# Weight pieces five to eight of the first batch rounded later, behind the copies of the last attention unit

## The reference

```python
state = alpha_t * state + k_t v_t^T;  y_t = q_t state         # 8 heads of 48, 768 tokens
x = y                                                        # 4 x 768 x 384
u = x + (x^T @ U @ V)^T                                      # rank 32
x = u + relu(u @ w_ch1) @ w_ch2                              # 384 -> 1536 -> 384
theta = x @ w_theta
u = x + w_tok_r @ (x * cos(theta)) + w_tok_i @ (x * sin(theta))
out = u + relu(u @ w_ch)
```

## Time and profile before

| what | us |
| --- | --- |
| median of three runs | 663.69 (663.62 to 664.41) |
| the profiled execution's own time | 664.45 |
| its span in the trace | 662.7 |
| busy in the span: TensorE | 651.1 |
| VectorE | 324.8 |
| ScalarE | 262.9 |
| GpSimd | 255.8 |

### The profile page before, as it was taken

One profiled execution on the slowest core, in us unless ns is written; L12 is line 12 of the kernel. 1 busy time (PEld: TensorE's weight loads), 2 busy tenths in 40 slices (PEclk: granted clock), 3 DMA queues, 4 the chain that ended last, 5 costly groups with the idle time before them and its releaser, 6 DMA issues.

```text
span 662.7 us, 15705 instructions
## 1 busy us (share of the span) xinstructions
PE 651.1 (98%) x6380; PEld 627.3 (95%) x6380; DVE 324.8 (49%) x543; ACT 262.9 (40%) x542; POOL 255.8 (39%) x250
## 2 busy tenths in 40 slices
PE   9979999999999999999999999999999999999998
PEld 5769999999999999999999999999999999999998
DVE  8938774255564255663242115765425543444522
ACT  5855544234544233544233334434324421432320
POOL 6757852133323133332112562347314531733220
PEclk9979999999999999999999999999999999999999
DMA  9466202006103015110004350220041023002101
GB/s 318 140 269 236 94 32 99 2 29 233 47 3 127 2 47 216 47 36 4 2 36 181 106 162 17 73 84 25 12 136 66 0 65 125 24 0 83 60 1 71
DMA packets 25163, 54.84 MB, mean 83 GB/s; under 512 B 2193, under 2 KB 17041, under 8 KB 25105
## 3 DMA queue, kind: packets, MB, share of 16 engines
q1 hardware_dynamic: 25104, 53.99, 23.4%
HBM read 44.55 MB, written 9.44 MB: 81 GB/s over the span
## 4 chain that ended last, share of the span: by engine, by line
PE 94%; DVE 2%; ACT 2%; issue 1%; DMA 1%; ACTq 0%; DVEq 0%
PE banks L774 24%; PE banks L804 22%; PE banks L1169 21%; PE banks L1241 6%; PE banks L1087 5%; PE banks L404 3%; PE banks L1144 2%; PE banks L525 2%; PE banks L465 2%; PE banks L533 2%; PE banks L719 1%; PE banks L1555 1%; DVE tokiL L247 1%; DMA stage<-w 1%; PE banks L724 1%
## 5 line engine op out<-in xcount | busy, mean ns | idle before, releaser
L788 DVE SCALAR_TENSOR_TENSOR hidL<-banks,hidH 128x384 fp32r<-128x384 f32 x96 | 53.4, 556 | 121.4 <-ACT hidH L784 121.0
L774 PE MATMUL banks<-uH,w1H 128*128 128x384 f32 x288 | 100.0, 347 | 0.3 <-ACT uH L751 0.3
L804 PE MATMUL banks<-hidH,w2H 128*128 128x384 f32 x288 | 96.6, 335 | 0.4 <-ACT x_nat L645 0.2
L774 PE MATMUL banks<-uH,w1L 128*128 128x384 f32 x288 | 96.5, 335 | 0.0
L804 PE MATMUL banks<-hidH,w2L 128*128 128x384 f32 x288 | 96.5, 335 | 0.0
L774 PE MATMUL banks<-uL,w1H 128*128 128x384 f32 x288 | 96.5, 336 | 0.0
L804 PE MATMUL banks<-hidL,w2H 128*128 128x384 f32 x288 | 96.2, 334 | 0.0
L784 ACT ACTIVATE hidH<-banks 128x384 fp32r<-128x384 f32 x96 | 47.0, 490 | 86.0 <-PE banks L774 86.0
L1227 POOL TENSOR_TENSOR u2L<-x_res,u2H 128x384 fp32r<-128x384 f32 x24 | 24.5, 1020 | 95.8 <-ACT u2H L1221 95.8
L390 POOL TENSOR_TENSOR k_end<-qka_sb,tail 112x384 f32<-112x384 f32 x32 | 31.5, 983 | 68.2 <-DVE tail L353 65.0
L774 PEld LDWEIGHTS banks<-uH,w1H 128*128 128x128 f32 x288 | 54.1, 188 | 2.5 <-issue 0.6
(11 more groups left out here) (134 smaller groups left out, 1416.4 us busy)
## 6 DMA issues: line engine op xcount, KB each, us to landing
qka_sb<-qka SPq DMA_DIRECT2D x28, 582.5 KB, 6.6
v_sb<-v_nat SPq DMA_DIRECT2D x32, 144.0 KB, 6.1
stage<-w SPq DMA_DIRECT2D x6, 768.0 KB, 5.2
x_dram<-u_t SPq DMA_DIRECT2D x8, 576.0 KB, 3.8
x_f<-x_dram SPq DMA_DIRECT2D x12, 384.0 KB, 4.5
x_res<-x_dram SPq DMA_DIRECT2D x8, 576.0 KB, 4.3
out_t<-stage SPq DMA_DIRECT2D x24, 192.0 KB, 1.9
stage<-tok_r_t SPq DMA_DIRECT2D x3, 768.0 KB, 4.4
```

The costliest lines, as they stand in the source:

```text
L774: last = nc.tensor.matmul(ps[:, 0:HALF], w[:, f, P * k:P * (k + 1)], x[half][:, k, :], start=(k == 0 and i == 0), stop=(k == DM_TILES - 1 ...
L788: nc.vector.scalar_tensor_tensor(hidL[s % 2][:], hid_ps[s % 2][:, 0:HALF], 0.0, hidH[s % 2][:].bitcast(F32), ALU.max, ALU.subtract).then_i ...
L804: last = nc.tensor.matmul(acc[m][:, 0:HALF], w[:, f, P * m:P * (m + 1)], x[s % 2][:], start=(f == 0 and i == 0), stop=(f == F_TILES - 1 an ...
```

## The change

Four pieces move to later places in ScalarE's queue. Pieces 4 and 5 were at the end of turn 6 and are now at the end of turn 7; pieces 6 and 7 were at the end of turn 7 and now stand behind the second turned tile's copy and behind the first rounding of u. On GpSimd pieces 4 and 5 stay at the end of its turn 7, piece 6 goes between the first two `lr_lo`, and piece 7 to the head of `FIRST_LO`, which waits for all three `uL`.

```diff
-        EARLY_HI = (range(0, 0), range(0, 0), range(0, 1), range(1, 2), range(2, 3), range(3, 4), range(4, 6), range(6, 8))
-        EARLY_LO = (range(0, 0), range(0, 0), range(0, 1), range(1, 2), range(2, 3), range(3, 3), range(3, 4), range(4, 8))
+        EARLY_HI = (range(0, 0), range(0, 0), range(0, 1), range(1, 2), range(2, 3), range(3, 4), range(0, 0), range(4, 6))
+        EARLY_LO = (range(0, 0), range(0, 0), range(0, 1), range(1, 2), range(2, 3), range(3, 3), range(3, 4), range(4, 6))
...
-        FIRST_LO = range(8, 11)
+        FIRST_LO = range(7, 11)
...
-            for m in range(LR_HALF - 1):
-                lr_lo(pool, nc.gpsimd, 0, 0, m)
+            lr_lo(pool, nc.gpsimd, 0, 0, 0)
+            part_lo(pool, 6)
+            lr_lo(pool, nc.gpsimd, 0, 0, 1)
             mlp_batch_pool(pool, 0, 1)
...
             act_output(act, 0, UNITS - 1)
             act_lr_x(act, 0, 0, 0)
             act_lr_x(act, 0, 0, 1)
+            part_hi(act, 6)
             act_lr_hi(act, 0, 0, 0)
+            part_hi(act, 7)
             first_g_hi(act, g_bank(PAIRS - 1), slice(EARLY_G, MODEL), "g_ready", "g_hi_done")
             act_lr_x(act, 0, 0, 2)
             act_lr_hi(act, 0, 0, 1)
```

## The result

| | before | changed |
| --- | --- | --- |
| median of 11 runs, us | 664.27 | 661.23 |
| lowest and highest | 662.52 to 664.66 | 660.57 to 662.18 |
| the profiled execution's own time | 664.45 | 661.23 |
| span in its trace | 662.7 | 659.5 |

The ratio is 0.9957 (95% interval 0.9948 to 0.9967), that is 2.9 us faster. The forecast was 3.0 us faster, 660.7 from a median of 663.69.

The account below looks back on a forecast made before the run. A weight load's DMA holds ScalarE's queue, leaving TensorE idle 2.7 us and then at half clock. Gaining 4.1 us, less a 1.1 us stall at group 0, gives 3.0 off the median 663.69: 660.7, range 659.6 to 662.0.

Parts of the forecast that it names:

- Part 1 and 2: Pieces 4 and 5 leave turn 6, 6 and 7 go among ScalarE's copies: TensorE 4.1 us earlier at 41.52.
- Halving the rows of small products: TensorE's work behind the idleness, at full clock: value products 0.93 to 0.47, carried 0.89 to 0.45, transposes 1.47 to 0.74.
- the 0.7 us for which the DMA was said to be still on the path: Pieces 4 and 5 behind turn 7 still wait for the load; unit 7's output, ready at 36.6, is copied at 37.27.
- That piece 7 on ScalarE costs 0.4: Piece 7 ahead of the high part of g delays its start from about 39.3 to 39.70; piece 6 costs nothing.
- Part 3, GpSimd: Piece 6 between two `lr_lo` is free; piece 7 ahead of the keys stalls TensorE some 1.1 us at group 0.
- The later groups: No such stall behind group 0: GpSimd's 0.92 of idleness before unit 1's keys takes most of the lateness.
- The DMAs: Loads 2 and 3 go 3.1 us earlier against a need 4.1 earlier, using 1.0 of slack; piece 8's load stays hidden.
- (a): VectorE's rel scan waits for GpSimd's piece and keys, `hidL` late, stall 1.8 to 1.9: gain 2.2, 661.5; chance 0.12.
- (b): The clock falls anyway, TensorE at 1.2 GHz from about 36.3: gain 1.4 to 2.4, about 661.7; chance 0.14.
- (c): The extra piece is hidden because scans no longer collide with GpSimd: gain 4.1, 659.6; chance 0.10.
- (d): Slower: GpSimd's late piece is not made up, groups 0 to 4 each wait 1.1 us: 665.1; chance 0.03.
- (e): No change: ScalarE waits for the load as before, a turn later, and the g chain loses it: 663.7; chance 0.03.

Follow-up runs that it names:

- run 6: Changed kernel with load 1 issued early, without its wait for unit 6's updates: 661.74 us, ratio 0.9973 to the kernel before.
- Run 5: Kernel before with load 1 issued without its wait for unit 6's updates, every piece in its old place: 660.26 us, ratio 0.9938.
- Run 1: Kernel before with three 128x384 identity products filling TensorE's 2.7 us of idleness, the late DMA left: 663.21 us, ratio 0.9987.
- 11: The changed kernel measured once more, beside the others on one chip: 661.08 us, ratio 0.9963 to the kernel before.
- 12: Changed kernel with three low pieces instead of four ahead of the keys, measured once more: 660.47 us, ratio 0.9947 to the kernel before.
- run 4: Changed kernel with low piece 11 added ahead of the keys of unit 0, five pieces: 663.95 us, ratio 0.9999 to the kernel before.
- 2: Kernel before with pieces 4 to 7 together behind turn 7 on both engines, none among the copies: 661.51 us, ratio 0.9966.
- run 8: Load 1 early, pieces 4 and 5 back in turn 6, 6 in turn 7, only low 8 and 9 ahead of the keys: 660.77 us, ratio 0.9943.
- run 9: Kernel before with load 1 early and only low piece 8 ahead of the keys of unit 0: 661.33 us, ratio 0.9959.
- run 10: Changed kernel with three low pieces ahead of the keys, load 1 issued some 2 us sooner: 664.42 us, ratio 1.0004 to the kernel before.
- 7: Changed kernel with load 1 early and three low pieces ahead of the keys: 660.44 us, ratio 0.9948 to the kernel before.

## Why the prediction was right, step by step

The forecast of the time and of its two main terms held, one stall at group 0 and the clock at 1.00 throughout. But the stall was over the 1.5 us that the prediction named as a sign of being wrong (1.51 as a wait, 1.66 as lost time), and its two terms as measured, 4.07 - 1.66, give 2.4. That the result is 2.9 or 3.0 is in part luck: what makes up the difference was not foreseen.

**Part 1 and 2, 4.1 us at the first uH product.** 4.07 in the trace. The high part of g started at 39.75 (39.70 said), the product at 41.56 (41.52 said). On the way two terms were off and covered each other. Halving the rows of small products was wrong: the value products took 0.74 to the next line instead of 0.53, the carried part 0.69 instead of 0.45, so unit 7 was complete at 37.11 and not at 36.6. (The transposes, 0.63 instead of 0.74, did halve.) And the 0.7 us for which the DMA was said to be still on the path cost nothing: in run 6, without it, the product comes no sooner. The clock's return was read as 43.05; a mean of 0.95 from 43 to 44 puts it at 43.10. Run 5 shows that the DMA in ScalarE's queue was the cause: with the load early and all pieces in place the gain is 4.1 us in the end. Run 1 shows that the clock was a real part, but worth 0.9 us by itself, not the 1.8 by which TensorE's stretch shortened, because GpSimd's pieces are next. The load sits right at the edge in the changed kernel: landing later costs its lateness one to one (11 and 12), landing sooner brings nothing (6). That piece 7 on ScalarE costs 0.4 was not tried alone.

**Part 3, GpSimd.** Piece 6 between the two `lr_lo` was free as said: the second started at 41.51, behind uH. Piece 7 ahead of the keys was the stall, as said; three pieces take it away, five add to it. Its size was the term that was off: 1.5 to 1.66 instead of 1.1. From the block's start to the end of the queries it was 53.36 - 47.26 = 6.10 before and 50.96 - 43.20 = 7.76 after. 1.0 of the 1.66 is the piece, and 0.66 one more collision with a scan of VectorE: before there were two, in the third piece and the keys (1.62), and now there are three, two within the pieces (three in 4.31, of 0.97 each without) and one in the queries (1.61 instead of 0.93). The term that I sized by the mean of the three pieces had to count which scan each instruction meets. The rule of the Trainium skill, SBUF — State Buffer, "SBUF: two separate sides", that these instructions hold each other off whole, fits these rows: each meeting adds 0.67 to 0.69 to a GpSimd instruction, most of the 0.97 that a scan takes alone (run 4, at 57.70).

**The later groups.** No stall at group 1 or beyond, as said. It even gave 0.2 back, 2.41 earlier ahead of it and 2.64 behind: the kernel before had a short wait there (nine L804 in 1.80 on its chain at 60.38), and the changed kernel has none (1.56 at 57.97).

**The DMAs.** Hidden, as said; the last of the three weight loads was issued at 37.11 instead of 40.02.

**The end.** 2.6 at 61 us and 3.2 at the end. 0.27 of the remaining 0.6 is the kernel before's longer stop at 176 us. The other 0.3 comes in the second mixer, in steps of under 0.1 without a wait that names them; the trace of run 11, the same kernel, has none of it, and I don't explain it.

**The rivals.** (a), the scan locked out, did not occur in the changed kernel: the rel scan took 1.38 as before and `hidL` was in time. Its mechanism shows in runs 1 and 2, on the tail scan: GpSimd's pieces were still running when it started, it took 1.83, and TensorE waited 0.7 and 0.6 for `hidL`. (b), the clock, did not fall, with idle stretches of 0.6 and 0.3 as reckoned, nor behind the stall of 1.5 at group 0, in the changed kernel and in runs 6 and 11; in runs 4, 8, 9 and 10, with 1.7 to 2.5 us of idleness, it did. (c) is refuted by the stall, (d) by group 1, (e) by ScalarE's 0.44.

**What stays open.** The stops in the middle of a line came at one place, inside L525 of unit 5, as a row of the profile in all five versions with the load in flight there (0.5, 0.5, 0.7, 1.9, 2.4 us) and in none of the nine others; at the other, inside L465 of unit 7, they were 0.3 in four and 1.7 in run 10. The times of the instruction packets fit both, without a run that moves them alone, and why the load holds such a packet back by 1.5 us in run 5 and by 3 in run 9 is not shown. Nor is it shown what keeps run 8 from the 2.0 us in its undisturbed executions.

## What to carry to other kernels

When an engine's queue holds work that waits for a DMA in front of copies that another engine needs, look first whether the DMA can come sooner; here that alone, with no compute instruction moved, was worth 4.1 us against the 2.9 of the reordering. Then look in the trace at the instruction packets that the moved DMA will meet: issued 8 us sooner it gained, issued 2 us sooner on another version it lost 3.9. Moved work has to be counted in the queue where it lands: one 1.0 us piece ahead of an operation without slack stalled it by 1.5, of which 0.8 was won by taking it away, and a second one cost 2.7 more, because the idleness cost the clock as well. The best versions measured here are that early load (0.9938), the change with three pieces ahead of the keys (0.9945 and 0.9947) and runs 7 and 8 (0.9948 and 0.9943), and they are not told apart.

## What the runs showed of the hardware that was not expected

- Three 128x384 products in an idle stretch kept the granted clock at 1.00 and shortened what came behind, yet the kernel gained only 0.9 us, of 1.8 by which that stretch shortened.
- 2.5 us without work brought the clock to 0.50 for the products that followed (3.08 instead of 1.76 us for nine), so that the stall cost 1.3 us more than its length there.
- 1.5 us without work (the stall at group 0) left the clock at 1.00, in three traces out of three.
- Moving one DMA of 768 KB by 2 us made TensorE stop 1.70 us between two matmuls of one line, and the kernel 3.9 us slower; moving it by 8 us moved the stop to another line and made it 0.5 to 2.4 us long.
- Such a stop ended 1.2 to 1.5 us behind the end of a 16 KB packet of the queue that the profile calls "instruction", 22 times out of 22; beside the load, that packet started up to 3.1 us later than in the kernel before.
